# One 128-row v tile for the last 64 tokens of two batches, and a convolution ring of three tiles in place of four

## The reference

```python
def _moe_ref(x, w_in, conv_w, w_out):
    h = np.maximum(x @ w_in, 0.0)                 # 512 -> 1024
    hp = np.concatenate([zeros, h, zeros], axis=1)    # one token at each end of a batch
    for k in range(3):
        conv_out += conv_w[k][None, None, :] * hp[:, k:k + S, :]
    gate = 1.0 / (1.0 + np.exp(-conv_out))
    return h * gate @ w_out                       # 1024 -> 512

def _moe2_ref(x, w_in, w_spatial, b_spatial, w_out):
    h = np.maximum(x @ w_in, 0.0)                 # 512 -> 1024
    u, v = (h[..., :d_ff // 2], h[..., d_ff // 2:])
    mu = np.mean(v, axis=-1, keepdims=True)
    var = np.mean((v - mu) ** 2, axis=-1, keepdims=True)
    v_n = (v - mu) / np.sqrt(var + 1e-06)
    v_s = np.einsum('ts,bsd->btd', w_spatial, v_n) + b_spatial[None, :, None]
    return (u * v_s) @ w_out                      # 512 -> 512
```

## Time and profile before

| | us |
|---|---|
| median of 3 runs | 513.01 (510.52 to 514.62) |
| profiled execution, its own time | 516.8 |
| profiled execution, span | 514.9 |
| TensorE busy, share of the span | 486.9, 95% |
| VectorE busy | 267.8, 52% |
| ScalarE busy | 254.5, 49% |
| GpSimd busy | 94.8, 18% |

### The profile page before, as it was taken

The page is one execution under the profiler, slowest core; times in us unless marked ns, Lnnn a source line. Parts: engine busy times, 40 slices in busy tenths (PEclk is TensorE's granted clock), DMA queues, the critical chain, the costliest instruction groups (busy, mean ns, idle before and its releaser), DMA issues.

```text
span 514.9 us, 9377 instructions
## 1 busy us (share of the span) xinstructions
PE 486.9 (95%) x3784; PEld 436.4 (85%) x3784; DVE 267.8 (52%) x482; ACT 254.5 (49%) x665; POOL 94.8 (18%) x159
## 2 busy tenths in 40 slices
PE   3668979999999999999999999999999999999997
PEld 2458969878888888877899979989998899989997
DVE  2539986497547946396349644834044503440040
ACT  2865865486538755486058474335213621262212
POOL 3638312241232221241003110001000100020000
PEclk9979979999999999999999999999999999999999
DMA  8961225201430312005000500001100010002002
GB/s 253 375 211 34 72 59 179 72 0 42 144 103 2 101 44 83 1 0 205 1 1 3 193 5 1 0 1 47 46 1 2 24 69 1 0 1 93 1 0 93
DMA packets 24223, 33.03 MB, mean 64 GB/s; under 512 B 1522, under 2 KB 13810, under 8 KB 24180
## 3 DMA queue, kind: packets, MB, share of 16 engines
q1 hardware_dynamic: 22324, 29.01, 17.1%
q10 hardware_dynamic: 1856, 3.42, 1.8%
HBM read 27.71 MB, written 4.72 MB: 63 GB/s over the span
## 4 chain that ended last, share of the span: by engine, by line
PE 82%; DVE 6%; DMA 4%; issue 3%; ACT 3%; POOL 1%; SPq 0%; ACTq 0%; DVEq 0%; POOLq 0%
PE dense L391 38%; PE pt_ps L391 10%; PE score L391 9%; PE pt_ps L586 6%; PE score L586 6%; DMA qk<-q_t 4%; PE x_ps L391 4%; PE x_ps L453 3%; PE pt_ps L437 3%; PE score L423 2%; DVE tmp L889 2%; DVE wr L874 1%; ACT vp L638 1%; PE score L416 1%; DVE ar L902 1%
## 5 line engine op out<-in xcount | busy, mean ns | idle before, releaser
L391 PE MATMUL dense<-xr,wr 128*128 128x512 f32 (+2 forms) x480 | 101.4, 371 | 3.3 <-POOL wr L1117 1.7
L391 PEld LDWEIGHTS dense<-xr,wr 128*128 128x128 f32 x480 | 87.8, 188 | 16.2 <-POOL wr L1117 2.0
L391 PE MATMUL dense<-ar,wr 128*128 128x512 f32 (+2 forms) x456 | 99.3, 374 | 0.3 <-DVE wr L874 0.3
L391 PEld LDWEIGHTS dense<-ar,wr 128*128 128x128 f32 x456 | 82.4, 188 | 11.5 <-DVE wr L874 0.6
L889 DVE SCALAR_TENSOR_TENSOR tmp<-tmp,taps 128x512 f32<-128x512 f32 (+2 forms) x80 | 57.7, 722 | 22.2 <-ACT tmp L679 20.7
L1111 POOL TENSOR_TENSOR vp<-vp,recip 128x1024 f32<-128x1024 f32 x18 | 34.5, 1917 | 108.3 <-DVE recip L853 108.3
L638 ACT ACTIVATE vp<-score,bias 128x128 f32<-128x128 f32 x128 | 45.0, 382 | 1.3 <-PE pt_ps L437 0.6
L1188 POOL TENSOR_TENSOR ident<-ident,minus_half 128x1 f32<-128x1 f32 (+1 forms) x20 | 11.0, 548 | 155.5 <-DVE ident L997 155.5
L671 ACT ACTIVATE tmp<-dense 128x512 f32<-128x512 f32 (+2 forms) x40 | 21.9, 549 | 34.0 <-PE dense L391 34.0
L805 ACT ACTIVATE ar<-vp 128x576 fp32r<-128x576 f32 x16 | 11.0, 687 | 50.1 <-DVE vp L1047 50.1
L391 PE MATMUL dense<-wr,xr 128*128 128x512 f32 x144 | 33.3, 389 | 0.0
(11 more groups left out here) (97 smaller groups left out, 752.2 us busy)
## 6 DMA issues: line engine op xcount, KB each, us to landing
vp<-v_rows SPq DMA_DIRECT2D x36, 256.0 KB, 4.0
out_t<-vp SPq DMA_DIRECT2D x16, 288.0 KB, 2.1
qk<-k_t SPq DMA_DIRECT2D x9, 384.0 KB, 3.8
qk<-q_t SPq DMA_DIRECT2D x9, 384.0 KB, 5.5
x2keep<-w_in ACTq DMA_DIRECT2D x2, 1024.0 KB, 11.0
qk<-w_in SPq DMA_DIRECT2D x1, 2048.0 KB, 9.6
x2keep<-w_out ACTq DMA_DIRECT2D x1, 1280.0 KB, 11.3
vp<-w_spatial_t SPq DMA_DIRECT2D x1, 1152.0 KB
```

The lines of the kernel that those rows point to most:

```text
L391: last = mm(dst, stationary(a, t), moving(c, t), start=(t == 0 and n == 0), stop=(t == of - 1 and n == 2))
```

## The change

Two things, the second to make room in on-chip memory for the first:

1. In the second part, s = 0 and 1, and s = 2 and 3, share a fifth v tile of 128 rows: rows 0 to 63 are the last 64 tokens of the even s, rows 64 to 127 those of the odd s. V_TILES is 5, 4, 5, 4 tiles. The tokens of the odd s are put behind those of the even one, in 64 further columns of `xt2`, by a new function `split_tail` on VectorE (two instructions over 4 x 64 columns, before `v_steps(0)` and before `v_steps(2)`). The normalised shared tile is kept in `v_tail` (in `prob_t`, which attention no longer needs), until the odd s has taken its rows too; the odd s puts high and low parts in the other halves of `vn`.
2. `conv` is a ring of three tiles, so tap0(n) waits for low(n-3) in place of low(n-4), in all five chunks of the first part.

```diff
-        xr = sb("xr", [P, 2 * KT * S], F32R)
+        xr = sb("xr", [P, 2 * KT * (S + TAIL)], F32R)
...
-        xt2 = [carve(xr, h * KT * S, KT, S) for h in range(2)]
+        xt2 = [carve(xr, h * KT * (S + TAIL), KT, S + TAIL) for h in range(2)]
...
-        tmp = sb("tmp", [P, 3 * (GW + 2) + 4 * GW], F32)
+        tmp = sb("tmp", [P, 3 * (GW + 2) + 3 * GW], F32)
...
-        conv = carve(tmp, 3 * (GW + 2), 4, GW)
+        conv = carve(tmp, 3 * (GW + 2), 3, GW)
...
+        v_tail = prob_t[:, 0:HEADS // 2, :].rearrange("p i n -> p (i n)")
...
+        V_TILES = [ST - s % 2 for s in range(B)]
+        V_AT = [sum(V_TILES[:s]) for s in range(B + 1)]
+        def v_normed(m):
+            return v_tail if m == ST - 1 else v_norm[:, m % 2, :]
...
             def v_tiles(s):
-                for m in range(ST):
-                    rows = P if m < ST - 1 else TAIL
+                for m in range(V_TILES[s]):
                     if s == 0 and m == 0:
                         pe.wait_ge(in2_lo, N_PIECES // 2)
...
                         pe.wait_ge(x2_lo, KT * s + KT)
                     if m == ST - 1:
-                        pe.wait_ge(v_relud, ST * s + 1)
+                        pe.wait_ge(x2_tail_lo, s // 2 + 1)
+                        pe.wait_ge(v_relud, V_AT[s] + 1)
                     elif s:
-                        pe.wait_ge(v_relud, ST * (s - 1) + (m + 1 if m else ST))
-                    last = product(v_bank(m)[0:rows, :], lambda a, t: xt2[a][:, t, m * P:m * P + rows],
+                        pe.wait_ge(v_relud, V_AT[s - 1] + (ST if m == 0 and s % 2 else m + 1))
+                    last = product(v_bank(m), lambda a, t: xt2[a][:, t, m * P:(m + 1) * P],
                                    lambda a, t: win2[a][:, t, G:2 * G], range(KT), KT)
                     last.then_inc(v_filled, 1)
...
-                        if n >= 4:
-                            act.wait_ge(gated_lo, n - 3)
+                        if n >= 3:
+                            act.wait_ge(gated_lo, n - 2)
                         act.wait_ge(carry_in, n + 1)
                         act.wait_ge(relu_done, n + 1)
-                        nc.scalar.activation(conv[:, n % 4, 0:W], h_pad[:, n % 3, 0:W], ACT.Copy,
+                        nc.scalar.activation(conv[:, n % 3, 0:W], h_pad[:, n % 3, 0:W], ACT.Copy,
...
+                for m in range(V_TILES[s] + 2):
+                    if m < V_TILES[s]:
+                        n = V_AT[s] + m
+                        if later(n - 2 if m >= 3 else V_AT[s]):
+                            act.wait_ge(vnorm_done, n - 2 if m >= 3 else V_AT[s])
...
+                        nc.scalar.activation(vn[0][0:rows, e, :], v_normed(e)[0:rows, :], ACT.Copy).then_inc(vn_hi, 1)
                     for i in extra[m:m + 1]:
                         late_high(i)
+                if s % 2:
+                    nc.scalar.activation(vn[0][TAIL:P, ST - 1, :], v_tail[TAIL:P, :], ACT.Copy).then_inc(vn_hi, 1)
...
+                for m in range(V_TILES[s] + 1):
+                    if m < V_TILES[s]:
+                        n = V_AT[s] + m
...
+                        if e == ST - 1:
+                            if s:
+                                dve.wait_ge(vn_tail_lo, s)
+                        elif later(free):
                             dve.wait_ge(vn_lo, free)
...
+                    if 2 <= m:
+                        v_low(s, m - 2)
                     for i in extra[m - 1:m] if m else ():
                         late_low(i)
+                if s % 2:
+                    v_low(s, ST - 2)
+                v_tail_low(s)
...
+            def v_tail_low(s):
+                mine, other = (slice(TAIL, P), slice(0, TAIL)) if s % 2 else (slice(0, TAIL), slice(TAIL, P))
+                dve.wait_ge(vnorm_done, V_AT[s - s % 2] + ST)
+                vec.tensor_copy(vn[1][0:TAIL, ST - 1, :], v_tail[mine, :])
+                dve.wait_ge(vn_hi, ST * s + ST)
+                vec.tensor_tensor(vn[0][other, ST - 1, :], v_tail[mine, :], vn[0][mine, ST - 1, :].bitcast(F32),
+                                  ALU.subtract).then_inc(vn_tail_lo, 1)
+            def split_tail(s):
+                at = SPAN * s + S - TAIL
+                kept = x2[:, :, at:at + TAIL]
+                vec.tensor_scalar(xt2[0][:, :, S:S + TAIL], kept, 1.0, None, ALU.mult).then_inc(x2_tail_hi, 1)
+                dve.wait_ge(x2_tail_hi, s // 2 + 1)
+                vec.tensor_tensor(xt2[1][:, :, S:S + TAIL], kept, xt2[0][:, :, S:S + TAIL].bitcast(F32), ALU.subtract
+                                  ).then_inc(x2_tail_lo, 1)
...
+            split_tail(0)
             v_steps(0, range(N_SPATIAL))
...
+                if s % 2:
+                    split_tail(s + 1)
                 v_steps(s + 1)
...
+                for m in range(V_TILES[s]):
+                    pool.wait_ge(vvar_done, V_AT[s] + m + 1)
+                    pl.tensor_tensor(vrstd[:, m:m + 1], vvar[:, m:m + 1], minus_half[:, :], ALU.pow
+                                     ).then_inc(vrstd_done, 1)
```

More of the change, by code:

```diff
@@ L212, in program @@
         x2last_lo = sem("x2last_lo")
+        x2_tail_hi = sem("x2_tail_hi")
+        x2_tail_lo = sem("x2_tail_lo")
         v_filled = sem("v_filled")
@@ L756, in v_steps @@
             def v_steps(s, extra=()):
[L758 to L764, removed]
+                for m in range(V_TILES[s] + 2):
[3 more added lines that the diff above has]
+                            act.wait_ge(vnorm_done, n - 2 if m >= 3 else V_AT[s])
                         act.wait_ge(v_filled, n + 1)
-                        nc.scalar.activation(v_relu[0:rows, m % 3, :], v_bank(m)[0:rows, :],
-                                             ACT.Relu, accum_out=vsum[0:rows, m:m + 1]).then_inc(v_relud, 1)
-                    if 1 <= m <= ST:
+                        nc.scalar.activation(v_relu[:, m % 3, :], v_bank(m), ACT.Relu,
+                                             accum_out=vsum[:, m:m + 1]).then_inc(v_relud, 1)
+                    if 1 <= m <= V_TILES[s]:
                         e = m - 1
[L770 to L777, removed]
+                        n = V_AT[s] + e
+                        if later(n):
+                            act.wait_ge(vsq_done, n)
+                        act.wait_ge(vmean_done, 2 * n + 1)
+                        nc.scalar.activation(v_junk, v_relu[:, e % 3, :], ACT.Square, bias=vmean[:, 0, e:e + 1],
+                                             accum_out=vsq[:, e:e + 1]).then_inc(vsq_done, 1)
                     if m >= 2:
@@ L893, in up @@
                         n = FT * c + f - 1
[L894 removed]
+                        y = conv[:, n % 3, 0:W]
                         dve.wait_ge(gate_done, n + 1)
@@ L982, in v_steps @@
             def v_steps(s, extra=()):
[L983 to L986, removed]
+                for m in range(V_TILES[s] + 1):
+                    if m < V_TILES[s]:
+                        n = V_AT[s] + m
                         dve.wait_ge(v_relud, n + 1)
                         for sign, value in enumerate((-1.0 / G, 1.0 / G)):
-                            vec.tensor_scalar(vmean[0:rows, sign, m:m + 1], vsum[0:rows, m:m + 1], value, None,
+                            vec.tensor_scalar(vmean[:, sign, m:m + 1], vsum[:, m:m + 1], value, None,
@@ L991, in v_steps @@
                                               ALU.mult).then_inc(vmean_done, 1)
-                    if 1 <= m <= ST:
+                    if 1 <= m:
                         e = m - 1
-                        rows = P if e < ST - 1 else TAIL
-                        dve.wait_ge(vsq_done, ST * s + e + 1)
-                        vec.tensor_scalar(vvar[0:rows, e:e + 1], vsq[0:rows, e:e + 1], 1.0 / G, 1e-6,
+                        n = V_AT[s] + e
+                        dve.wait_ge(vsq_done, n + 1)
+                        vec.tensor_scalar(vvar[:, e:e + 1], vsq[:, e:e + 1], 1.0 / G, 1e-6,
@@ L998, in v_steps @@
                                           ALU.mult, ALU.add).then_inc(vvar_done, 1)
-                        n = ST * s + e
                         free = (ST - 1) * s + (e - 1 if e >= 2 else 0)
-                        if later(free):
+                        if e == ST - 1:
+                            if s:
+                                dve.wait_ge(vn_tail_lo, s)
+                        elif later(free):
                             dve.wait_ge(vn_lo, free)
                         dve.wait_ge(vrstd_done, n + 1)
-                        vec.tensor_scalar(v_norm[0:rows, e % 2, :], v_relu[0:rows, e % 3, :],
-                                          vmean[0:rows, 1, e:e + 1], vrstd[0:rows, e:e + 1],
+                        vec.tensor_scalar(v_normed(e), v_relu[:, e % 3, :], vmean[:, 1, e:e + 1], vrstd[:, e:e + 1],
@@ L1024, in v_steps, with v_low @@
                     for i in extra[m - 1:m] if m else ():
                         late_low(i)
+                if s % 2:
+                    v_low(s, ST - 2)
+                v_tail_low(s)
```

(6 more changed lines are left out.)

33 lines of the change are left out of this document (7 added, 26 removed).

## The result

The changed kernel takes 537.33 us (median of 4 runs, 536.34 to 539.92) against 513.74 (510.52 to 514.62): ratio 1.047, 95% interval 1.0434 to 1.0506. It is slower by 23.6 us; forecast were 23.7. Its profiled execution took 536.34 us with a span of 534.6 and a mean granted clock of 0.971.

A forecast was written before the change was run, and what follows sets the result against it. TensorE was taken as the bound, except chunk 0's convolution and exponentials, with no slack for a slower convolution. Gain -4.3, ring +20.5 and clock +7.5 make +23.7: 536.7 us, range 525 to 541.5.

The forecast's parts named there:

- The gain, 4.3: Second part: 24 matmuls fewer save 5.5 us, less 1.2 of longer waits: 4.3 us faster, bounds 3.9 and 5.5.
- the late copy on ScalarE: Third tile of out(0): first copy only 2.0 to 2.4 us earlier; wait grows 0.6 us in each odd s.
- `split_tail` cost nothing: Before the v steps of s = 0 and 2: hidden; if that cover were gone, 0.84 us twice.
- The loop: Convolution: period 3.53 us instead of 2.66; 4.3 us per 512-column chunk, 3.8 per 384-column chunk; 20.5 us slower in all.
- One bound of the prediction: Upper bound on the ring's cost: 25 us if handovers cost 0.2 each in place of 0.03.
- No slack behind it: Chunks 1 and 2: exponentials and TensorE's work arrive together, so the convolution's delay lands fully, 4.3 us each.
- Chunk 4: Its third down piece waits for relu(7), which moves by the loop's delay: 3.8 us or a little more.
- The clock, 7.5: Stops in chunks 1 to 3 bring TensorE's clock down: three falls of 2.5 us, 7.5 slower, bounds 0 and 10.
- rival B: The clock falls in chunk 4 too: +26.2, 539.2 us; chance 0.20.
- Rival A: The ring costs what was forecast, but the clock holds: +16.2, 529.2 us; chance 0.20.
- Rivals C: Delay partly absorbed in one or two chunks: half the ring's cost and one clock fall, +8, 521 us; chance 0.07.
- D: Faster: tap0's wait for low(n-3) is covered and only the gain is left, 508.7 us; chance 0.03.

The follow-up runs named there:

- the pairing alone: Kernel before plus the shared v tiles, convolution ring kept at four tiles, extra x columns in the fourth tile of vn: 509.15 us, ratio 0.9898.
- two strict tiles: Kernel before, ring of four kept, tap0(n) waiting for low(n-3) only in the last two tiles of each chunk: 521.91 us, ratio 1.0159.
- the fill for chunks 1 and 2: Changed kernel plus 12 unused matmuls ahead of the second attention step in chunks 1 and 2: 535.05 us, ratio 1.0406 to the kernel before.
- three strict tiles: Kernel before, ring of four kept, tap0(n) waiting for low(n-3) only in the last three tiles of each chunk: 530.06 us, ratio 1.0326.
- five strict tiles: Kernel before, ring of four kept, tap0(n) waiting for low(n-3) for f >= 3 of each chunk: 542.05 us, ratio 1.054.

## Why the prediction was right

The sign, the place and the size held. That the totals agree to 0.1 us is luck: the four runs of the changed kernel alone spread over 3.6 us. Term by term:

- **The gain, 4.3.** Measured 4.32 in the second part's stretch, and 4.5 by the runs of the pairing alone. The 1.2 us that I took off the 5.5 for the late copy on ScalarE is 2 x 0.60 in the chain (20.03 to 17.87 us from v(1) to the third tile of out(0), where 2.76 went), and an edit at that very place gave it back. `split_tail` cost nothing that can be seen; nor did its four-instruction form in the pairing with a ring of four.
- **The loop.** Period 3.53 us, measured 3.53; 4.3 us for a chunk of 512 columns, measured 4.26, 4.17 and 4.31; 3.8 for chunk 0, measured 3.84. This is why the handover was taken from the row and not at 0.60 us from start to start: by the rule of the Trainium skill ("VectorE: DVE Perf Modes", "The DRAIN you can't avoid"), read over to two engines, the period would have been 3.41 (an estimate, 3.53 - 0.12); the trace has 119.54 to 120.26, 0.72 us, between the starts of low and tap0. The page speaks of instructions of one engine, and there (gate to low, 0.60) it is not contradicted. One bound of the prediction was added up wrongly: two handovers in each of 25 iterations, at 0.2 us in place of 0.03, make 20.5 + 25 x 0.34 = 29 us and not 25. No run came near either.
- **No slack behind it.** The exponentials arrived together with TensorE (0.18 us ahead of it in chunk 1), so nearly each microsecond of the loop landed. The strict tiles show it for every length: stops of 1.54, 2.43 and 4.20 us in chunk 1 for 2, 3 and 5 of them.
- **Chunk 4.** The third piece waits for relu(7), as forecast, and the second for relu(6): stops of 2.12 and 1.11 us, forecast 2.4 and 1.4. That stretch lost 5.28 us, of which 13.48 - 66 x 12.92/72 = 1.6 is the clock, so the loop's part is 3.6 (forecast 3.8).
- **The clock, 7.5.** Right in sum, not in its parts. Forecast were three falls at 2.5 us; measured were four, at 2.40, 1.24, 2.73 and 1.6, together 8.0. The term that was mis-sized is the price of one fall: three at 2.5 were to cost 7.5 in chunks 1 to 3 and cost 6.4, and chunk 4 was put at nothing. Chunk 4 was called against (rival B had 0.20, and its mechanism is what happened), and the price taken from one row held for one chunk of the two that were like it. That the two errors cancel is luck. In chunk 0 the step behind the old stop became 0.43 us shorter.

Rival A (the clock holds) is what the kernel with two strict tiles shows in chunks 1 to 4, for stops of 1.16 to 2.88 us; the changed kernel lost its clock in all four. Rivals C and D (something absorbs the delay) find no support in any run.

That the low clock and not something else makes the steps behind a stop slow is shown by the fill for chunks 1 and 2. For chunks 3 and 4 it rests on the windows and on the same pattern; no run filled those stops.

## What to carry to other kernels

A ring of n tiles between two engines is a number in a sum: write down the cycle from the release of a tile to its next release, and compare it with the period of the slower engine. Here the fourth tile kept a 0.7 us step on ScalarE out of VectorE's cycle, 2.66 us against 3.53; the tile cost 2 KB in each partition, and as much room as the change needed could be found in a buffer that is idle at that time. Then look for who arrives together with the slowed chain before counting on slack, and count what the tensor engine may lose in clock as well: here a stop of 2.0 us brought it down once and left it alone three times. An edit that takes work off the bounding engine also moves forward what that engine waits for next: moving one copy ahead brought the missing part of the gain.

## What the runs showed of the hardware

The length of a stop alone did not decide whether the clock fell. Stops of 1.45, 1.54 and 1.94 us left it alone, and so did those of 2.00 and 2.01 us (changed kernel and filled stops, chunk 0), of 1.99 us (three strict tiles, chunk 0) and of 2.88 us (two strict tiles, chunk 3). Stops of 2.33 and 2.43 us (three strict tiles) brought it down, and so did one of 2.02 us (five strict tiles, chunk 0): the three matmuls behind that one took 1.29 us at a granted clock of 0.55, where they took 0.80 behind the stop of 2.00 us. The pair of 1.11 (1.12) and 2.12 us in chunk 4, with three matmuls between, brought it down each of the three times that it came (changed kernel, filled stops, five strict tiles).

It could fall after the work had resumed. Behind the 2.43 us stop the clock was 1.00 to its end and at 0.88 over the first microsecond of work. With five strict tiles the same stop in chunk 1 lasted 4.20 us, and the clock outlasted it too (windows over the second half of the stop and the work behind it):

```profile
128.50:130.70 2.20, 0.00 (x0) 1.00 0.00 0
130.70:134.00 3.30, 3.26 (x62) 0.57 0.00 0
```

And how much a fall cost lay between 1.24 and 2.73 us in one execution, by when the clock fell and rose again. An estimate for one stop from one row is good to about a factor of two; only the sum over several was good here.
